# Second layer: matmuls of a product and of two output units take turns one by one in four slots of seven

## The reference, cut to what matters

```python
def reference(q, k, v, f, moe_w_in, moe_w_out, moe2_w_in, moe2_w_out):
    x = attention_with_decay(q, k, v, f)      # 4 x 8 heads, 576 rows, 64 wide -> x: 2304 x 512
    h = x @ moe_w_in                          # 512 x 2048
    g = np.maximum(h, 0.0) ** 2
    x = g @ moe_w_out                         # 2048 x 512
    h = x @ moe2_w_in
    g = np.where(h >= 1, h, np.where(h <= -1, 0.0, (h + 1) ** 2 / 4))
    return g @ moe2_w_out
```

## Time and profile before

| | |
|---|---|
| median of 3 runs | 963.64 us (963.54 to 965.24) |
| the profiled execution's own time | 962.2 us |
| its span | 960.4 us |
| TensorE (PE) busy | 948.4 us, 99% of the span |
| VectorE (DVE), ScalarE (ACT) busy | 631.2 us, 646.5 us |
| GpSimd (POOL) busy | 154.4 us, all in the attention |
| granted TensorE clock | 0.999 of full speed |

### The profile page before, as it was taken

How to read it: one execution, slowest core, us unless ns; L and a number is a source line. 1 busy time by engine, 2 the same in 40 slices (tenths; PEclk the granted TensorE clock), 3 DMA queues, 4 the chain that set the end, 5 groups by cost and what they waited for, 6 DMA issues and landing times.

```text
span 960.4 us, 16613 instructions
## 1 busy us (share of the span) xinstructions
PE 948.4 (99%) x5554; PEld 861.9 (90%) x5554; DVE 631.2 (66%) x1286; ACT 646.5 (67%) x1345; POOL 154.4 (16%) x204
## 2 busy tenths in 40 slices
PE   9999999989999999999999999999999999999998
PEld 8888888879999999999999999989888998888987
DVE  7888898996666544346444488778765565755554
ACT  6888888886666756557655577666765566655564
POOL 7777898700000000000000000000000000000000
PEclk9999999999999999999999999999999999999999
DMA  7445454155556552524344235545654525353401
GB/s 225 154 149 170 147 170 148 58 181 194 172 190 251 199 183 114 198 104 193 122 174 145 98 95 191 192 170 209 262 198 164 198 99 197 120 201 143 195 23 67
DMA packets 61942, 155.13 MB, mean 162 GB/s; under 512 B 4624, under 2 KB 28688, under 8 KB 61872
## 3 DMA queue, kind: packets, MB, share of 16 engines
q1 hardware_dynamic: 61872, 154.23, 45.1%
HBM read 120.06 MB, written 34.15 MB: 161 GB/s over the span
## 4 chain that ended last, share of the span: by engine, by line
PE 96%; DVE 2%; ACT 1%; issue 1%; POOL 0%; ACTq 0%; POOLq 0%
PE banks L1404 36%; PE banks L1449 21%; PE banks L1441 14%; PE banks L1443 7%; PE banks L1353 6%; PE banks L1298 5%; PE banks L1308 4%; PE banks L1324 1%; PE banks L1366 1%; DVE rsum L1059 1%; PE banks L1357 1%; DVE pT L1034 0%; DVE h_tile L1156 0%; ACT pr L825 0%; PE banks L1349 0%
## 5 line engine op out<-in xcount | busy, mean ns | idle before, releaser
L1404 PE MATMUL banks<-xs,wi_hi 128*128 128x384 f32 x1344 | 343.2, 336 | 2.9 <-DVE h_tile L1156 2.0
L1404 PEld LDWEIGHTS banks<-xs,wi_hi 128*128 128x128 f32 x1344 | 235.9, 188 | 25.6 <-issue 3.2
L1404 PE MATMUL banks<-xs,wi_lo 128*128 128x384 f32 x672 | 225.4, 335 | 0.0
L1449 PE MATMUL banks<-wo_hi,gs 128*128 128x512 f32 x576 | 205.6, 393 | 0.0
L1441 PE MATMUL banks<-gs,wo_hi 128*128 128x512 f32 x384 | 141.6, 391 | 0.2 <-DVE gs L1170 0.2
L923 ACT ACTIVATE gs<-h_tile 128x384 fp32r<-128x384 f32 x192 | 100.6, 525 | 60.2 <-DVE h_tile L1165 57.0
L899 ACT ACTIVATE s_tile<-banks 128x384 f32<-128x384 f32 x144 | 70.0, 487 | 90.0 <-PE banks L1404 90.0
L1170 DVE TENSOR_TENSOR gs<-h_tile,gs 128x384 fp32r<-128x384 f32 x192 | 106.5, 555 | 35.4 <-ACT gs L923 32.6
L1404 PEld LDWEIGHTS banks<-xs,wi_lo 128*128 128x128 f32 x672 | 126.2, 188 | 0.0
L1449 PEld LDWEIGHTS banks<-wo_hi,gs 128*128 128x128 f32 x576 | 108.1, 188 | 17.6 <-DVE gs L1170 0.2
L1449 PE MATMUL banks<-wo_lo,gs 128*128 128x512 f32 x288 | 113.8, 395 | 0.0
(11 more groups left out here) (107 smaller groups left out, 1444.8 us busy)
## 6 DMA issues: line engine op xcount, KB each, us to landing
wi_hi<-kept_weights SPq DMA_DIRECT2D x32, 896.0 KB, 5.6
wi_lo<-kept_weights SPq DMA_DIRECT2D x32, 896.0 KB, 7.4
wo_raw<-moe_w_out_dram SPq DMA_DIRECT2D x48, 512.0 KB, 4.0
kept_weights<-wi_hi SPq DMA_DIRECT2D x16, 896.0 KB, 6.2
kept_weights<-wi_lo SPq DMA_DIRECT2D x16, 896.0 KB, 8.0
qk_raw<-qk_dram SPq DMA_DIRECT2D x15, 608.0 KB, 6.4
wi_raw<-moe_w_in_dram SPq DMA_DIRECT2D x32, 256.0 KB, 7.5
cb<-cum_scratch SPq DMA_DIRECT2D x30, 256.0 KB, 4.1
```

The costliest lines, as they stand in the source:

```text
L1404: last = mm(ps, w[a][:, W_OF[i], t * P:(t + 1) * P], xs[i][:, b, t, :], start=(i in (0, 1, 2, 5) and t == a == b == 0), stop=(i in (0, 3, ...
L1449: last = mm(banks[:, t, n0:n1], gs[:, q % 2, jj, a, t * P:(t + 1) * P], w[b][:, jj, n0:n1], start=(fresh and a == b == 0), stop=(done and ...
```

## The change

Four things. In `group`, where the units belong to the second layer and the group is not the first of its chunk, products 1, 2, 3 and 4 (`PAIRED`) are issued by a new function `both`: after each matmul of the product comes one of a unit, so that the six of the product and the six of two units take turns. `per_slot` becomes [0, 2, 2, 2, 2, 3, 1] for the second layer: product 0 has no unit behind it, product 5 has three. `ACT_GROUP` and `DVE_GROUP`, which hold for both layers, are written in a new order. The rest only splits functions (`product_waits`, `product_mm`, `unit_waits`, `place_of`, `unit_mm`, `last_unit`). The number of matmuls, their operands and the data moved stay.

```diff
-    ACT_GROUP = [("G", 3), ("X", 0), ("K", 3), ("x", 6), ("C", 0), ("C", 1), ("H", 0), ("Y", 0), ("H", 1),
-                 ("W", 0), ("C", 2), ("X", 1), ("X", 2), ("X", 3), ("Y", 1), ("G", 0), ("K", 0), ("G", 1),
-                 ("K", 1), ("G", 2), ("Y", 2), ("X", 4), ("K", 2), ("X", 5)]
-    DVE_GROUP = [("G", 3), ("Q", 0), ("x", 5), ("K", 3), ("X", 0), ("x", 6), ("A", 0), ("H", 0), ("H", 1),
-                 ("W", 0), ("X", 1), ("A", 1), ("Y", 0), ("G", 0), ("A", 2), ("X", 2), ("K", 0), ("G", 1),
-                 ("A", 3), ("X", 3), ("Y", 1), ("K", 1), ("Z", 0), ("G", 2), ("A", 4), ("Y", 2), ("K", 2),
-                 ("X", 4)]
+    ACT_GROUP = [("G", 3), ("X", 0), ("x", 6), ("C", 0), ("K", 3), ("C", 1), ("H", 0), ("Y", 0), ("H", 1),
+                 ("W", 0), ("X", 1), ("Y", 1), ("C", 2), ("X", 2), ("X", 3), ("G", 0), ("K", 0), ("G", 1),
+                 ("Y", 2), ("X", 4), ("K", 1), ("G", 2), ("K", 2), ("X", 5)]
+    DVE_GROUP = [("G", 3), ("x", 5), ("Q", 0), ("X", 0), ("K", 3), ("A", 0), ("x", 6), ("H", 0), ("H", 1),
+                 ("W", 0), ("X", 1), ("A", 1), ("X", 2), ("Z", 0), ("G", 0), ("A", 2), ("Y", 0), ("K", 0),
+                 ("G", 1), ("A", 3), ("X", 3), ("Y", 1), ("K", 1), ("G", 2), ("A", 4), ("X", 4), ("Y", 2),
+                 ("K", 2)]
...
+    PAIRED = (1, 2, 3, 4)
...
-        return [1, 1, 1, 1, 1, 1, 2] if layer_of(q) == 0 else [2, 2, 1, 2, 2, 2, 1]
+        return [1, 1, 1, 1, 1, 1, 2] if layer_of(q) == 0 else [0, 2, 2, 2, 2, 3, 1]
...
+            def both(q, i, n):
+
+                product_waits(q, i)
+                for t in range(2):
+                    unit_waits(q - 1, n + t)
+                    for a, b in TERMS:
+                        product_mm(q, i, t, a, b)
+                        unit_mm(q - 1, n + t, a, b)
...
                 for i in range(PRODUCTS_W):
+                    if layer_of(q - 1) and q % GROUPS_W and i in PAIRED:
+                        both(q, i, n)
+                        n += 2
+                        continue
                     product(q, i)
                     for _ in range(per_slot(q - 1)[i]):
                         unit(q - 1, n)
```

## The result

The changed kernel takes 968.87 us in the median of 6 runs (968.02 to 970.78), beside 964.06 us for the kernel before on the same chip: a ratio of 1.0057, 95% interval 1.0046 to 1.0068. It is slower, by 4.8 us; I had forecast 962.8 and "no change" as the likeliest.

What follows compares the result with a forecast made beforehand. TensorE, busy 99%, was taken to bound the kernel through matmul pace and rare waits. Terms: -2.5 (turned groups) + 1.05 (product 5) + 0.4 (split of x) + 0.25 (last units) = -0.8 us, giving 962.8; 8-in-10 range 959.7 to 967.6.

Steps and rivals of the forecast that it cites:

- the turns: Second-layer slots where product and unit matmuls alternate: 2.40 us a slot against 2.43 before, bounds 2.40 to 2.58.
- rival 4: Each return trip between 384 and 512 columns costs 0.01 to 0.03 us: total 967 to 977 us; chance 0.14.
- Product 5's wait: Second-layer product 5's weight load, released by smooth 0, comes 0.12 us late: 0.05 us a group, +1.05 us in all.
- Rival 3: Product 5's wait becomes the bound, 0.25 us a group: total 967.1 us, slower; chance 0.12.
- The split of units and the orders: New ScalarE and VectorE orders move work within idle stretches, free; no new wait expected at product 1.
- The last units: At the kernel's end, combine 2 and all behind it sit 0.2 us later: +0.25 us, bounds 0 to 0.4.
- Product 6 and the first layer: Product 6's cover by combine 3 just holds, no wait; first-layer groups keep their pace, 0, at most +0.5 us.
- Rival 1: Second layer's whole excess over the quiet pace goes and product 5's wait costs nothing: -4.2 us, 959.5; chance 0.18.
- Rival 2: Mixing order is worth nothing: second-layer groups stay at 15.69 us and the waits add, total 964.5 us; chance 0.14.

Runs made afterwards that it cites:

- PPUU: Changed kernel with the order of a turned slot's twelve matmuls varied by group, group 34 having two product, two unit matmuls, three times: a middle slot loses 80 ns.
- The widths: Changed kernel, and one without turns, with second-layer units of 128 to 512 columns by group: turned slots lose 0 ns at 384 columns, 80 at 512.
- the first layer's runs: Kernel before with first-layer units issuing three 512-column matmuls, then three of 256, not in turn: groups 15.853 instead of 15.600 us; one execution 967.33 beside 963.99.
- turns of three: Changed kernel with three product matmuls, then three of a unit, twice in a slot: 965.31 us beside 963.89 before, ratio 1.0016.
- the kernel with runs by group: Kernel before, nothing turned, with second-layer units spread over slots differently in each group: two layers' stretch 756.41 us beside 745.66.

## Why the prediction was wrong

The step that failed is the first of the working, **the turns**: "I take 2.40." It measured 2.469 for the first slot of a group and 2.480 for the three others, against 2.434 before. I had put the four slots at 9.62 us; they take 9.91, so 0.29 more a group and 6.1 us more in 21 groups, which alone turns my -0.8 into +5.3. Against the kernel without turns (2.430 to 2.434 for the same slots) they are 0.18 us longer in a usual group. The bounds (2.40 to 2.58) held the slot, and rival 4 ("each turn costs", a slot 0.03 to 0.15 longer, chance 0.14) named the time that came: its total started at 967, and 968.87 lies in it but outside my range, which left most of that rival out. Its mechanism, a price for each return trip, came out only in part: six trips a slot (PU) and three (PPUU) lose the same 80 ns, and six trips lose 0 with units of 384 columns. I chose the end of the bounds by one row group, in which turns of 512 and 256 columns are quiet, and carried it to turns of 384 and 512. The widths and the first layer's runs show that such a row doesn't carry to other lengths.

The other steps, against the stretch:

- *Product 5's wait*: I had 0.05 a group. It measured 0.03 in most groups (0.203 against 0.174 us for the first matmul) and 0.05 in three; the longer slot 4 gives the chain more time, as the working said it would: in group 33, with slots of 2.44, it is 0.08. In groups 31 and 39, with the split of x ahead of gate 0, it is 0.14 more; I had 0.2. Rival 3 falls. The working took 0.15 us from the release of a load to its matmul, and product 5 in group 31 shows the same; the late load in the last units, below, shows 0.05.
- *The split of units and the orders*: the orders are free, as said. The split costs 0.76 us in groups 25, 33 and 41, and 0.56 in all; product 1's wait there was not in my sum.
- *The last units*: I had +0.25, it measured +0.21 (8.25 us from the first start of group 47's units to the last, against 8.04); the other 0.20 of the 0.41 from group 47 on are its own turned slots. The changed kernel's late load, against the earlier trace rows, and the split that released it:

```profile
958.07 0.19 PEld L1489 LDWEIGHTS banks<-wo_hi,gs 128*128 128x128 f32 x1 [0.46 <-DVE gs L1171]
...
957.46 0.56 DVE L1171 TENSOR_TENSOR gs<-h_tile,gs 128x384 fp32r<-128x384 f32 x1
```

- *Product 6 and the first layer*: product 6 has no new wait and first-layer groups take 15.600, as said.

Together, read slot by slot against the kernel without turns: 3.57 us for the four turned slots in 21 groups (0.19 of it is product 5 starting late in groups 31 and 39), 0.79 for product 5 and the three units behind it, 0.28 for the last units (8.25 against 7.97) and 0.04 elsewhere, 4.68; with 0.55 for the split without turns, 5.23.

Rival 1 (the whole excess goes) falls with the slots at 2.48. Rival 2, "order is worth nothing", falls with turns of three, of one and none at 15.734, 15.887 and 15.680 us. The Trainium skill ("TensorE: Matmul & The Clock Gate", Back-to-back issue gap) gives columns over 2.4 GHz and 2.5 ns for the gap of a matmul by itself, 216 ns at 512 columns, and for a stream in which each matmul has its weight load about 131 ns at 512 columns. The traces agree with neither: with a weight load at each matmul a long run goes at 226.7 ns.

What stays open is what the matmul meets. Shown: it is a loss of pace without a wait; it depends on the lengths of the neighbours and not on which tiles are held or moved; turns over the same banks and semaphores lose nothing where both have 384 columns; within a group it repeats to the ns; in a run of equal matmuls it dies out within about ten; in turns of one it stays, at 40 or 80 ns a slot by how the turns are entered. That weight loads and streams fall into unlucky phases fits all of it, but no run shows the mechanism.

## What to carry to other kernels

Where TensorE is busy 99%, read the pace from start to start and compare it with the pace of a long run of equal matmuls: what lies between the two is the most that a new order can give, here 0.25 us of 15.7. Take that pace from a run of the very length: here no one formula gave it for all. An order that is quiet for one pair of lengths says nothing of another pair; measure the very mixture, several variants in one kernel by group, before building a schedule on it. And an order that only takes away spacing between a result and its next use has a price in the first groups and the last units, where no steady state covers it.

## What the runs showed of the hardware

- A matmul of 384 or 512 columns with its own weight load costs columns / 2.4 GHz + 13.3 ns in a long run of its kind, 173.3 and 226.7 ns; at 448, 464, 480 and 496 columns it is 3 to 7 ns more than that (207, 210, 217 and 223 ns), and at 128 columns 111 ns. After a change between 384 and 512, up to nine matmuls run 1 to 12 ns off, in a fixed pattern.
- Matmuls of 384 and 512 columns in turn go at 0.413 or 0.406 us a pair, the same code in the same kernel, by how the turns were entered (groups 41 and 33 of the changed kernel).
- In the kernel with runs by group product 6 of group 37 waited 1.86 us; 1.5 us after it had started again the granted clock was 0.50 for 3.2 us, the lower level of 1.2 GHz. There a matmul of 384 columns took 0.32 us, so 384 / 1.2 GHz and nothing on top. Behind the other wait of that length, in group 44, matmuls of 384 and 512 columns took 0.320 and 0.427 us for a while. The first, its stretch and then its rows:

```profile
798.10:801.30 3.20, 3.20 (x12) 3.20 (x11) 1.93 (x5) 2.17 (x5) 0.00 (x0) 0.50 0.74 262
```

```profile
796.47 0.61 PE L1407 MATMUL banks<-xs,wi_hi 128*128 128x384 f32 x2 [1.86 <-DVE h_tile L1159]
...
799.01 0.53 PE L1407 MATMUL banks<-xs,wi_lo 128*128 128x384 f32 x1
799.33 0.53 PE L1407 MATMUL banks<-xs,wi_hi 128*128 128x384 f32 x1
```

- A weight load released late starts its matmul 0.05 us after the release (958.02 to 958.07 in the changed kernel's last units, and product 6 in the runs by group), but 0.15 in the first group of a chunk and at product 5 in groups 25 and 31 of the changed kernel; the matmul behind it comes 0.08 to 0.11 us late as well.
- Executions of one kernel differ by some 3 us, and in these profiles it lies in the attention: the kernel before and the one with the new orders alone have spans of 960.4 and 963.6 us, with group 1 starting at 211.2 and 214.4 and a stretch of 745.66 and 745.65.
